# Fused attention and two MLPs on one core: the scan's preparation with carries by pairs, two pieces handed to ScalarE, and a later place for its first steps

## The reference

```python
# q, k, v, a_re, a_im: (4, 8, 768, 48)
mag = np.sqrt(a_re * a_re + a_im * a_im)
scale = np.minimum(mag, 0.999) / (mag + 1e-06)
a_re_n, a_im_n = (a_re * scale, a_im * scale)
for t in range(S):
    ar, ai = (a_re_n[:, :, t, :, None], a_im_n[:, :, t, :, None])
    new_re = ar * S_re - ai * S_im
    new_im = ar * S_im + ai * S_re
    S_re, S_im = (new_re + kv(t), new_im)            # kv(t) = k_t outer v_t
    y[:, :, t] = np.einsum('bhd,bhde->bhe', q[:, :, t], S_re)
# x: (3072, 384) from y; w_in (384, 2048), w_out (2048, 384)
h = x @ w_in
x = (np.maximum(h, 0.0) + np.log1p(np.exp(-np.abs(h)))) @ w_out
# w1, w2 (384, 1024), w3 (1024, 1024), w_out2 (1024, 384)
out = ((x @ w1) * (x @ w2)) @ w3 @ w_out2
```

## Time and profile before

| | before |
|---|---|
| median of 3 runs | 982.48 us (980.43 to 983.35) |
| profiled execution | 982.79 us, its span 981.0 us |
| TensorE busy | 920.0 us, 94% of the span |
| VectorE busy | 599.0 us, 61% |
| ScalarE busy | 436.1 us, 44% |
| mean granted TensorE clock | 0.974 of full |
| chain that ended last | PE 67%, DVE 17%, ACT 5%, DVE queue 4%, DMA 3% |

### The profile page before, as it was taken

How to read it: one execution, slowest core, us unless ns; L and a number is a source line. 1 busy time by engine, 2 the same in 40 slices (tenths; PEclk the granted TensorE clock), 3 DMA queues, 4 the chain that set the end, 5 groups by cost and what they waited for, 6 DMA issues and landing times.

```text
span 981.0 us, 14349 instructions
## 1 busy us (share of the span) xinstructions
PE 920.0 (94%) x5352; PEld 811.1 (83%) x5352; DVE 599.0 (61%) x976; ACT 436.1 (44%) x619; POOL 70.5 (7%) x58
## 2 busy tenths in 40 slices
PE   4995939999999999999999999999999999999998
PEld 1554839989989989989899999999788888888887
DVE  4968678989898998898999832355221212121211
ACT  5262254585674674664764654587102020202011
POOL 0000000000000000000000000000222222222221
PEclk9997669999999999999999999999999999999999
DMA  9477066273372391480570550421101010101000
GB/s 336 181 213 237 20 194 134 78 195 91 109 173 83 109 220 38 141 210 14 157 195 13 143 114 14 147 90 46 36 1 65 1 64 1 64 0 64 0 33 33
DMA packets 97878, 99.50 MB, mean 101 GB/s; under 512 B 6928, under 2 KB 88848, under 8 KB 97808
## 3 DMA queue, kind: packets, MB, share of 16 engines
q1 hardware_dynamic: 97808, 98.59, 34.8%
HBM read 63.96 MB, written 29.88 MB: 96 GB/s over the span
## 4 chain that ended last, share of the span: by engine, by line
PE 67%; DVE 17%; ACT 5%; DVEq 4%; DMA 3%; issue 3%; SPq 1%; ACTq 1%
PE ps_p L1345 7%; PE ps L1345 7%; PE ps L1347 7%; PE ps L1346 7%; PE ps_p L1347 7%; PE ps_p L1346 7%; PE ps_ay L1407 4%; DVE sp L1223 2%; PE ps_ay L1347 2%; PE ps_ay L1346 2%; PE ps_ay L1345 2%; DMA w3s<-in_w3t 2%; PE ps_k L1347 2%; PE ps_k L1345 2%; PE ps_k L1346 2%
## 5 line engine op out<-in xcount | busy, mean ns | idle before, releaser
L1345 PE MATMUL ps<-g_h,wo_h 128*128 128x384 f32 x384 | 132.8, 346 | 2.2 <-DVE g_l L1230 2.2
L666 POOL TENSOR_TENSOR abl<-ab,abh 128x512 fp32r<-128x512 f32 x48 | 69.1, 1440 | 903.4 <-DVE abh L1328 903.4
L1347 PE MATMUL ps<-g_h,wo_l 128*128 128x384 f32 x384 | 129.1, 336 | 0.0
L1346 PE MATMUL ps<-g_l,wo_h 128*128 128x384 f32 x384 | 128.8, 335 | 0.0
L1345 PE MATMUL ps_p<-x1h,win_h 128*128 128x384 f32 x336 | 116.8, 348 | 6.0 <-DVE sp L1223 6.0
L1347 PE MATMUL ps_p<-x1h,win_l 128*128 128x384 f32 x336 | 112.6, 335 | 0.0
L1346 PE MATMUL ps_p<-x1l,win_h 128*128 128x384 f32 x336 | 112.5, 335 | 0.0
L1319 DVE TENSOR_TENSOR ab<-ps_ay,bc 128x512 f32<-128x512 f32 x24 | 16.6, 692 | 114.1 <-ACT bc L953 114.1
L775 ACT ACTIVATE sp<-ps_p 128x768 f32<-128x768 f32 (+1 forms) x63 | 46.2, 733 | 86.2 <-PE ps_p L1347 86.2
L788 ACT ACTIVATE g_h<-sp 128x768 fp32r<-128x768 f32 (+1 forms) x71 | 55.3, 779 | 65.0 <-DVE sp L1223 64.6
L1319 DVE TENSOR_TENSOR ab<-ps_p,bc 128x512 f32<-128x512 f32 x24 | 16.6, 692 | 103.1 <-ACT bc L953 103.1
(11 more groups left out here) (167 smaller groups left out, 2037.0 us busy)
## 6 DMA issues: line engine op xcount, KB each, us to landing
qk_scr<-tt SPq DMA_DIRECT2D x16, 576.0 KB, 5.4
stq<-qk_scr SPq DMA_DIRECT2D x48, 192.0 KB, 4.8
qk_scr<-pp SPq DMA_DIRECT2D x16, 576.0 KB, 4.2
stk<-qk_scr SPq DMA_DIRECT2D x48, 192.0 KB, 4.6
an<-in_a_re SPq DMA_DIRECT2D x8, 576.0 KB, 4.1
an<-in_a_im SPq DMA_DIRECT2D x8, 576.0 KB, 5.5
qk<-in_q SPq DMA_DIRECT2D x8, 576.0 KB, 7.7
qk<-in_k SPq DMA_DIRECT2D x8, 576.0 KB, 9.3
```

What stands on the lines that cost most here:

```text
L666: tensor_tensor(abl[:, m % AR, :], ab[:, m % 2, :], abh[:, m % AR, :].bitcast(F32), ALU.subtract).then_inc(ab_lo, 1)
L1345: mm(o, wh, xh, start=start, stop=False)
L1346: mm(o, wh, xl, start=False, stop=False)
L1347: return mm(o, wl, xh, start=False, stop=stop)
```

## The change

For tiles 2 to 7 the change does this.

- **Carries by pairs.** `carry in` multiplies the odd carries with their even neighbours (24 pairs a group), `carry` runs on the pairs with distances 1, 2, 4, 8, 16, and `carry out` multiplies the even ones with the pair before them: seven steps of 144, 138, 132, 120, 96, 48 and 138 elements for six of 282, 276, 264, 240, 192 and 96. All tiles have this. They are also spread in another way over steps 2 and 3.
- **Run ends by ScalarE.** ScalarE copies the run ends (`prep_ends`), in step 2 behind the outputs' copy and ahead of the softplus of step 3; it waits for run 7, and VectorE waits for it before `carry in`.
- **r - 1e6 by ScalarE.** `prep_scale_start` is gone. ScalarE makes r - 1e6 (`prep_root_less`) behind the Newton step and the softplus of step 0, ahead of its high part; `prep_scale` takes the minimum and the product in one operation and waits for it. In tiles 0 and 1 VectorE makes r - 1e6.
- **Squares and root behind high parts.** On ScalarE the squares of tile n + 3 move behind the high part of step 6, the logarithm behind the softplus of step 7 and root and its square behind that step's high part. On VectorE m2 moves from step 5 behind `x1_low` of step 6, Newton behind `g_low` of step 7, scale behind `add_relu` of step 0.
- **The inverse in two.** Its first multiply stands ahead of the mask of step 5, the second behind it.

```diff
+            def prep_ends(m):
+                carries = gp[:, :, :].rearrange("p c (g r) -> p c g r", g=G)
+                ends = an[:, :, :].rearrange("p c (g k i r) -> p c g k i r", g=G, i=RUN, r=CR)
+                most = (NCH - 1) * CR
+                eng.wait_ge(runs_made, m + 1 - IN_SLOTS)
+                for c in range(2):
+                    act(carries[:, c, :, 1:1 + most].rearrange("p g (k r) -> p g k r", r=CR),
+                        ends[:, c, :, 0:NCH - 1, RUN - 1, :], ACT.Copy)
+                act(carries[:, :, :, 1 + most:NR], ends[:, :, :, NCH - 1, RUN - 1, 0:CR - 1], ACT.Copy).then_inc(ends_out, 1)
+
+            def prep_root_less(m):
+                eng.wait_ge(prep_root_made, m + 1 - IN_SLOTS)
+                act(te[:, 0, :], te[:, 1, :], ACT.Copy, bias=-1e6).then_inc(prep_less, 1)
...
                         y_out(n + 1, j - 1)
                     if has_prep and j == 5:
                         prep_inverse(n + 2)
+                    if has_prep and j == 2:
+                        prep_ends(n + 2)
...
-                        if nxt_prep and j == 5:
-                            prep_squares(n + 3)
                         g_high(n, j + 1, split)
                     elif j == NP1 - 2:
                         if nxt_prep:
-                            prep_log(n + 3)
-                            prep_root(n + 3)
+                            prep_squares(n + 3)
                         if nxt:
                             for part in range(2):
                                 y_loaded(n + 1, part)
                                 x1_high(n + 1, part)
+                        softplus(n, j + 1, split)
                         if nxt_prep:
-                            prep_root_square(n + 3)
-                        softplus(n, j + 1, split)
+                            prep_log(n + 3)
                         g_high(n, j + 1, split)
+                        if nxt_prep:
+                            prep_rsqrt(n + 3)
                     elif nxt:
                         softplus(n + 1, 0, False)
+                        if nxt_prep:
+                            prep_root_less(n + 3)
                         g_high(n + 1, 0, False)
...
-            def prep_scale_start(m):
-                ve.tensor_scalar(tr[:, :], te[:, 1, :], 0.999, 1.0, ALU.mult, ALU.min)
-                eng.drain()
 
             def prep_scale(m):
-                ve.scalar_tensor_tensor(out=tr[:, :], in0=te[:, 1, :], scalar=-1e6, in1=tr[:, :],
-                                        op0=ALU.add, op1=ALU.mult)
+                if m < IN_SLOTS:
+                    ve.tensor_scalar(te[:, 0, :], te[:, 1, :], -1e6, None, ALU.add)
+                    eng.drain()
+                else:
+                    eng.wait_ge(prep_less, m + 1 - IN_SLOTS)
+                ve.scalar_tensor_tensor(out=tr[:, :], in0=te[:, 1, :], scalar=1.0 / 0.999, in1=te[:, 0, :],
+                                        op0=ALU.min, op1=ALU.mult)
                 eng.drain()
...
+            def prep_carry_in():
+                t = gp[:, :, :].rearrange("p c (a l) -> p c a l", l=2)
+                n = GC * CR // 2
...
+                cmul(t[:, 0, :, 1], t[:, 1, :, 1], t[:, :, :, 0],
+                     t[:, 0:1, :, 1].to_broadcast([P, 2, n]), t[:, 1:2, :, 1].to_broadcast([P, 2, n]), m1, m2)
...
-            before_mask = {0: steps("a", 1), 1: steps("run", 3, 4), 2: steps("run", 7) + ["ends"] + steps("carry", 1),
-                           3: steps("carry", 8, 16, 32), 4: by[3:] + ["p"], 5: []}
-            after_mask = {0: steps("run", 1), 1: steps("run", 5), 2: steps("carry", 2), 3: by[:2], 4: [("q", 0)], 5: ["inverse"]}
-            after_sum = {0: steps("run", 2), 1: steps("run", 6), 2: steps("carry", 4), 3: by[2:3], 4: [("q", 1), "p2"], 5: ["keys"]}
+            before_mask = {0: steps("a", 1), 1: steps("run", 3, 4), 2: steps("run", 7) + ["ends", "carry in"],
+                           3: steps("carry", 8, 16) + ["carry out"], 4: by[3:] + ["p"], 5: ["inverse start"]}
+            after_mask = {0: steps("run", 1), 1: steps("run", 5), 2: steps("carry", 1), 3: by[:2], 4: [("q", 0)], 5: ["inverse end"]}
+            after_sum = {0: steps("run", 2), 1: steps("run", 6), 2: steps("carry", 2, 4), 3: by[2:3], 4: [("q", 1), "p2"], 5: ["keys"]}
...
                     if nxt_prep and j == 6:
-                        prep(n + 3, not even, ["newton"])
+                        prep(n + 3, not even, ["m2"])
                     if j < NP1 - 1:
                         add_relu(n, j + 1, split)
                     elif nxt:
+                        add_relu(n + 1, 0, False)
                         if nxt_prep:
                             prep(n + 3, not even, ["scale"])
-                        add_relu(n + 1, 0, False)
                     if has_prep and j < 6:
                         prep(n + 2, even, after_sum[j])
-                    if nxt_prep and j == 5:
-                        prep(n + 3, not even, ["m2"])
-                    if nxt_prep and j == 6:
-                        prep(n + 3, not even, ["scale start"])
                     if j < NP1 - 1:
                         g_low(n, j + 1, split)
                         if has_prep and j == 5:
                             prep(n + 2, even, ["keys end"])
+                        if nxt_prep and j == 6:
+                            prep(n + 3, not even, ["newton"])
```

More of the change, by code:

```diff
@@ L1022, in prep_run, with prep_carry_start @@
                      ms[:, 2 * GC * CR:4 * GC * CR].rearrange("p (c a r) -> p c a r", c=2, a=GC))
-            def prep_carry_start(even):
+                if i == RUN - 1 and m >= IN_SLOTS:
+                    last.then_inc(runs_made, 1)
+            def prep_carry_start(m, even):
                 if even:
@@ L1036, in prep_carry_start @@
-                eng.drain()
+                if m < IN_SLOTS:
+                    ends = an[:, :, :].rearrange("p c (g k i r) -> p c g k i r", g=G, i=RUN, r=CR)
+                    most = (NCH - 1) * CR
+                    for c in range(2):
+                        ve.tensor_copy(carries[:, c, :, 1:1 + most].rearrange("p g (k r) -> p g k r", r=CR),
+                                       ends[:, c, :, 0:NCH - 1, RUN - 1, :])
+                    ve.tensor_copy(carries[:, :, :, 1 + most:NR], ends[:, :, :, NCH - 1, RUN - 1, 0:CR - 1])
+                else:
+                    eng.wait_ge(ends_out, m + 1 - IN_SLOTS)
@@ L1105, in prep @@
                         prep_newton(m)
-                    elif piece == "scale start":
-                        prep_scale_start(m)
                     elif piece == "scale":
@@ L1112, in prep @@
                     elif piece == "ends":
[L1113 removed]
+                        prep_carry_start(m, even)
                     elif piece == "p":
@@ L1119, in prep @@
                         prep_p2_(m)
-                    elif piece == "inverse":
-                        prep_inv_newton(m)
+                    elif piece == "inverse start":
+                        prep_inv_start(m)
+                    elif piece == "inverse end":
+                        prep_inv_end(m)
                     elif piece == "keys":
@@ L1190, in _ @@
             tokens_mask()
[L1191 to L1193 removed]
+            prep(0, True, ["m2", "newton", "scale"] + steps("a", 0, 1) + steps("run", 1, 2, 3, 4, 5, 6, 7) +
+                 ["ends"] + ["carry in"] + steps("carry", 1, 2, 4, 8, 16) + ["carry out"] + by + ["p", ("q", 0), ("q", 1), "p2", "inverse start", "inverse end", "keys", "keys end"], first=True)
+            prep(1, False, ["m2", "newton", "scale"] + steps("a", 0, 1))
             prep(1, False, steps("run", 1, 2, 3, 4, 5, 6, 7))
             raw_low(6)
[L1196 removed]
+            prep(1, False, ["ends", "carry in"])
             mask_scores(0, 0)
[L1198 removed]
+            between = [steps("carry", 1), steps("carry", 2), steps("carry", 4), steps("carry", 8), steps("carry", 16) + ["carry out"],
                        by[:1], by[1:2], by[2:3], by[3:], [], ["p"], []]
@@ L1209, in _ @@
             x1_low(0)
-            prep(1, False, ["p2", "inverse", "keys", "keys end"])
+            prep(1, False, ["p2", "inverse start", "inverse end", "keys", "keys end"])
             prep(2, True, ["m2"])
```

64 lines of the change are left out of this document (39 added, 25 removed).

## The result

The change takes 999.07 us in the median (995.98 to 1002.71, 4 runs) against 982.91 (980.43 to 983.50, 4 runs): a ratio of 1.0163, 95% interval 1.0136 to 1.0191. The forecast was 987.0 with a range of 976 to 993. The direction was right and the size was not.

The account below looks back on a forecast made before the run. It took TensorE to wait only for VectorE in the slots, some 11.5 us. Terms 3.2 + 1.45 + 0.5 - 0.4 = +4.7 us on 982.8 (profiled) or 982.5 (median) gave 987.5 or 987.2; likeliest 987, range 976 to 993.

Parts of the forecast that it names:

- Slot ends, +3.2 us: Ends of slots 0 to 4: small waits gather into one before step 0's result matmuls; odd +0.35, even +0.85 us each.
- nearly on time: Slot ends: the next tile's score matmuls would start almost unwaited, with add 0 falling at 14.6 to 15.6 us.
- the squares before x1h fit into the 2.52 us that ScalarE idles there: Slot end on ScalarE: squares ahead of x1_high fill existing idle time of 2.52 us, as read from slot 5.
- r - 1e6 on ScalarE: Slot-end chain: ScalarE needs 1.16 us against VectorE's 0.75; staying on VectorE would shorten each of five chains by 0.5 us.
- Inverse in two, +1.45: Step 5: the mask between the multiplies delays add 6 by 0.6 us in three even slots, less 0.35 in slot 2.
- run ends, +0.5: Steps 2 and 3: ScalarE's copies and hand-overs cost between 0 and 0.5 us a slot, taken as 0.17.
- Carries by pairs, 0: Steps 2 and 3: VectorE saves 1.1 us a slot, which buys it idle time and TensorE nothing.
- Start, -0.4: Before the first mask: tile 1's ends and first carry shrink from 1.49 to 1.06 us, within TensorE's wait of 8.78 us.
- Rival 3: Slot ends: 3 us holes halve TensorE's clock, up to 3.1 us longer matmuls five times; chance 0.10 shared with another rival.

Follow-up runs that it names:

- the hold of four: Kernel before plus four useless VectorE multiplies ahead of g_low of step 0 at the ends of slots 0 to 4: 1003.62 us, ratio 1.0218.

## Why the forecast was wrong in size

1. *Slot ends, +3.2 us.* Right in the mechanism: U7, D6, U0 and U1 follow each other without a wait (but one of 0.2 us), and the waits gather behind them. They are in two pieces and not in the one of 2.9 to 3.2 us that was forecast: 0.33 to 1.11 us ahead of the first scores, which were to be "nearly on time", and 2.2 us ahead of D0. Slots 0 and 1 came to 0.08 us of the forecast. Measured +5.67 us. The missing 2.5 us are mostly the transfer of y (1.18 + 0.90 + 0.24 = 2.3 by the waits), which the step "the squares before x1h fit into the 2.52 us that ScalarE idles there" did not ask about: I took the start of x1h from slot 5, where y was there in time, and did not say what became of the cover when logarithm and root left. This is read from the timelines; no variant takes the wait for y out by itself.
2. *r - 1e6 on ScalarE.* The forecast held that "rows agree" with the Trainium skill's rule (ScalarE: Activation LUTs, Rules for kernel authors) that adds and multiplies belong on VectorE, and put 0.5 us a chain on it. The order printed ahead of the prediction shows why: the operation needs only Newton, as add 0 needs only the softplus, so the two run side by side. Taken alone the operation is shorter on VectorE, as the rule has it: 0.75 us against 1.17 by the timelines above. In this chain the measurement decides against the rule: VectorE's version made it 0.63 us longer.
3. *Inverse in two, +1.45, and run ends, +0.5.* Together 1.95, measured 1.46 in the rest of the slots. U7 of slot 0 waits 1.16 us for add 6, 0.56 before, which is the 0.6 us of the forecast. Taken apart by the variants' traces, the split costs 0.9 us (409.5 to 408.6) and the run ends 0.4 (408.6 to 408.2), one trace each; in the times neither can be told from nothing (ratios 1.0011, 1.0001 and 1.0006).
4. *Carries by pairs, 0.* Right: the carry operations of all eight tiles took 63.0 us before and 55.1 after, 1.0 us less a tile where 1.1 was forecast, and the time did not follow (ratio 1.0006 with the pairs and r - 1e6 on ScalarE alone). The rest of VectorE's fall from 599.0 to 583.3 us is r - 1e6 and the run ends.
5. *Start, -0.4.* The wait it names went from 8.78 to 8.34 us, as forecast. What that gives to the whole is not measurable beside the 3.1 us by which executions differ there.
6. *The clock.* This is the step that failed: the sum takes D0 behind the new hole at its old length, so the clock stands in it at nothing. Rival 3 named it, with its place and its price: "with 2 us each it is 997". It happened at all five ends of the profiled execution, 1.9 us each (9.47 us in all). It had less than 0.10 of the chances and stood outside the range, and the prediction gives no reason for that. It cites one hole, of 12.60 us. Its own rows have a second, of 8.78 us, behind which eight scores took 2.08 us, also at half speed. The trace of before has a third, of 5.83 us (at 127.15), with the granted clock at 0.50 behind it. And it has one of 2.37 us, ahead of the product of w3 and w_out2, behind which 32 matmuls ran as fast as the same 32 did later in an unbroken stretch:

```profile
23.86 10.59 PE L1373 MATMUL ps_p<-wo2s,w3s 128*128 128x384 f32 x32 [2.37 <-DMA w3s<-in_w3t]
...
53.02 10.48 PE L1373 MATMUL ps_p<-wo2s,w3s 128*128 128x384 f32 x32
```

   So before showed holes of 5.83 us and more with half speed behind them and one of 2.37 without. The forecast holes of 2.9 to 3.2 us lay between, nothing in the rows spoke for either side, and the range should have held both. The measured holes of 2.2 us are shorter than the harmless one, and the clock fell all the same.

   The Trainium skill says that idle gaps put the array back to its lower clock (TensorE: Matmul & The Clock Gate, HAM oscillation); the traces agree, in the change and with the hole made on purpose, and filling the hole undoes it.

My sum with the right price for that step is 4.7 + 9.5 = 14.2 us above 982.8, which is 997.0; with the 2.5 us for y it is 999.5, and the median is 999.07. These are the same numbers put together afterwards, no second forecast.

## What to carry to other kernels

A wait that is gathered is not the same as a wait that is spread: the same idle time in one piece can take TensorE's clock with it, and then costs more in matmuls at half speed: 9.5 us beside 11.2 us of waits ahead of D0 in the change, 7.3 beside 12.9 in the hold of four. Before moving work so that small waits merge into one, look in the trace at hand for holes of that length and at the speed behind them. One harmless hole is one case and no promise: 2.37 us before and 2.50 us in one slot of the hold cost nothing, and 2.24 us in the change cost the clock five times. Where the rows do not settle it, the range must hold both prices. And when an operation leaves a place on an in-order engine, ask for each one behind it what it had been covering, transfers above all.
